# First stage in nine groups of tokens, three of 256 and six of 384; the lead needs two blocks of 128; idle products in the lead

## What is computed

```python
for t in range(S):                                   # stage 0, S = 768, D = 48
    cur = np.einsum('bhd,bhe->bhde', u[None] * kt, vt)
    y[:, :, t] = np.einsum('bhd,bhde->bhe', rt, state + cur)
    state = wt[:, :, :, None] * state + np.einsum('bhd,bhe->bhde', kt, vt)
...
h = x @ w_in                                         # first dense stage, 384 -> 2048 -> 384
g = np.where(pos, h, np.where(neg, 0.0, (h + beta) ** 2 / (4.0 * beta)))
x = g @ w_out
...
silu = g * (1.0 / (1.0 + np.exp(-g)))                # second dense stage, 384 -> 1536 -> 384
out = silu * (x @ w_val) @ w_out
```

## Time and profile before

| | us |
|---|---|
| median of 3 runs | 966.13 (965.5 to 968.37) |
| profiled execution, its time | 966.24 |
| its span, first to last instruction | 964.5 |
| PE busy (9142 products) | 947.0 |
| DVE busy | 519.5 |
| ACT busy | 402.5 |
| POOL busy | 164.2 |

### The profile page before, as it was taken

The page is one execution under the profiler, slowest core; times in us unless marked ns, Lnnn a source line. Parts: engine busy times, 40 slices in busy tenths (PEclk is TensorE's granted clock), DMA queues, the critical chain, the costliest instruction groups (busy, mean ns, idle before and its releaser), DMA issues.

```text
span 964.5 us, 22023 instructions
## 1 busy us (share of the span) xinstructions
PE 947.0 (98%) x9142; PEld 928.7 (96%) x9142; DVE 519.5 (54%) x909; ACT 402.5 (42%) x845; POOL 164.2 (17%) x155
## 2 busy tenths in 40 slices
PE   6899999999999999999999999999999999999998
...
DMA packets 23511, 61.96 MB, mean 64 GB/s; under 512 B 2688, under 2 KB 12032, under 8 KB 23424
## 3 DMA queue, kind: packets, MB, share of 16 engines
...
## 4 chain that ended last, share of the span: by engine, by line
PE 94%; DVE 3%; issue 1%; ACT 1%; DMA 1%; SPq 0%; DVEq 0%; ACTq 0%
PE bank L1254 50%; PE bank L1282 35%; PE bank L1313 2%; PE bank L1337 2%; PE bank L1332 2%; PE bank L1302 1%; PE bank L1343 1%; DMA w_by_channel<-in_w_channel 1%; PE bank L1324 1%; DVE suf L1000 1%; DVE gate L1104 0%; DVE glo L1097 0%; DVE k_r_by_channel L1025 0%; PE bank L1299 0%; ACT state_decayed L806 0%
## 5 line engine op out<-in xcount | busy, mean ns | idle before, releaser
L841 ACT ACTIVATE ghi<-gate 128x384 fp32r<-128x384 f32 x224 | 117.2, 523 | 184.9 <-DVE gate L1116 95.4
L1097 DVE TENSOR_TENSOR glo<-gate,ghi 128x384 fp32r<-128x384 f32 x224 | 133.5, 596 | 106.3 <-ACT ghi L841 104.0
L1114 DVE TENSOR_TENSOR gate<-bank,gate 128x384 f32<-128x384 f32 x96 | 53.5, 558 | 215.0 <-ACT gate L960 215.0
L1254 PE MATMUL bank<-xhi,w2gv_ahi 128*128 128x384 f32 x480 | 161.3, 336 | 0.0
L1254 PE MATMUL bank<-xlo,w2gv_ahi 128*128 128x384 f32 x480 | 161.3, 336 | 0.0
L1254 PE MATMUL bank<-xhi,w2gv_alo 128*128 128x384 f32 x480 | 161.3, 336 | 0.0
L960 ACT ACTIVATE gate<-bank 128x384 f32<-128x384 f32 x96 | 47.2, 492 | 227.7 <-PE bank L1254 227.7
L1282 PE MATMUL bank<-ghi,w1ohi 128*128 128x384 f32 x384 | 133.9, 349 | 0.9 <-DVE glo L1097 0.9
L1254 PE MATMUL bank<-xhi,w1ihi 128*128 128x384 f32 x384 | 129.2, 337 | 2.1 <-DVE gate L1104 1.2
L1282 PE MATMUL bank<-glo,w1ohi 128*128 128x384 f32 x384 | 129.2, 336 | 0.0
L1254 PE MATMUL bank<-xhi,w1ilo 128*128 128x384 f32 x384 | 129.1, 336 | 0.0
...
## 6 DMA issues: line engine op xcount, KB each, us to landing
...
```

The source lines that it names most:

```text
L841: e.activation(ghi[j % 2][:, :], gate[j % 2][:, :], ACT.Copy).then_inc(M["hi", ph], 1)
L1097: e.tensor_tensor(glo[j % 2][:, :], gate[j % 2][:, :], ghi[j % 2][:, :].bitcast(F32), ALU.subtract)\
L1114: e.tensor_tensor(q, hid[j % 2][:, 0:T], q, ALU.mult).then_inc(M["t", 2], 1)
L1254: m = e.matmul(out, w_of(a, k), x_of(b_, k), start=start and i == 0, stop=stop and i == total - 1)
```

## The change

The first stage is worked in nine groups: three of two windows (256 tokens), then six of three (384 tokens). The second stage keeps its eight groups of 384. In the first three groups, each product of the first stage has 256 columns instead of 384, and so have the gate's instructions on ACT and DVE; the number of products in a group stays at 288. The lead has two windows instead of three; the third window's pieces move into the slots of group 0. Groups of two windows have slot tables of their own, and windows are counted through from 0 to 23, so the three buffers of r, k, v and w are used in turn over group borders. The transfers of the lead stand in another order: window 2's come behind the first weight chunks. DVE forms the rests of seven chunks (0, 1, 3, 7, 13, 19, 25) instead of one. In the lead, idle products of 128x256 stand in PE's list (five ahead of KT of window 0, on a tile of zeros; three on constants ahead of KT of window 1, three ahead of Y of window 0) in place of the twelve transposes. The result of a group of 256 is stored in one or two pieces.

```diff
+SIZES = (2, 2, 2, 3, 3, 3, 3, 3, 3)
+NG1 = len(SIZES)
+BASE = [sum(SIZES[:g]) for g in range(NG1 + 1)]
+ROW = S // WIN
+PIECES = 6
...
 FIRST_FILLS = [("KT", 0, 0), ("AT", 0, 0), ("AT", 0, 1), ("ST", 0, 0),
                ("KT", 1, 0), ("AT", 1, 0), ("AT", 1, 1), ("Y", 0, 0),
-               ("ST", 1, 0), ("KT", 2, 0), ("AT", 2, 0), ("AT", 2, 1),
-               ("Y", 1, 0), ("Y", 2, 0), ("XT", 0, 0), ("XT", 1, 0), ("XT", 2, 0), ("ST", 2, 0)]
-
-WARM = 12
+               ("Y", 1, 0), ("XT", 0, 0), ("XT", 1, 0), ("ST", 1, 0)]
+FIRST_BANKS = (0, 1, 2, 3, 4, 5, 6, 7, 0, 1, 3, 2)
+IDLE = {("KT", 0): 5, ("KT", 1): 3, ("Y", 0): 3}
+
...
-XT_FIRST = 13
+
+
+def visits_at(n, slots):
+    return {j: tuple(FILLS[n].index(f) for f in visit) for j, visit in zip(slots, VISITS[n])}
+
+
+WIN_SLOTS = {2: visits_at(2, (3, 5, 7, 9, 11)), 3: visits_at(3, (3, 5, 6, 8, 9, 11, 12))}
+WIN_FIRST = visits_at(2, (4, 6, 8, 10, 12))
+XT_FIRST = 12
...
-CHECK_FIRST = {0: 1, 3: 2}
-SCAN_FIRST = {1: 1, 5: 2}
-SCALE_FIRST = {0: 0, 2: 1, 8: 2}
-DIAG_FIRST = {2: 0, 5: 1, 7: 2}
-SCAN_SLOTS_FIRST = {11: 0, 14: 1, 15: 2}
-
-
-DVE_CHUNK = 3
+CHECK_FIRST = {0: 1}
+SCAN_FIRST = {1: 1}
+SCALE_FIRST = {0: 0, 2: 1}
+DIAG_FIRST = {3: 0, 7: 1}
+SCAN_SLOTS_FIRST = {11: 0, 14: 1}
+
+
+DVE_CHUNKS = (0, 1, 3, 7, 13, 19, 25)
+DVE_CHUNK_SLOTS = {1: 7, 4: 13, 7: 19, 10: 25}
 HI_FIRST = {0: 13, 1: 13, 2: 15, 3: 18, 4: 21, 5: 24, 6: 27, 7: 30, 8: 32}
-PRODUCTS_AT = {10: 0, 17: 1, 22: 2}
-VALUES_AT = {16: 0, 23: 1, 28: 2}
+PRODUCTS_AT = {5: 0, 14: 1}
+VALUES_AT = {12: 0, 20: 1}
 
...
+def no(g, w):
+    return BASE[g] + w
+
+
+def place_of(n):
+    g = max(g for g in range(NG1) if BASE[g] <= n)
+    return g, n - BASE[g]
+
+
 def win_slots(g):
-    return WIN_FIRST if first(g) else WIN_SLOTS
+    return WIN_FIRST if first(g) else WIN_SLOTS[SIZES[g + 1]]
...
+        def width(ph, g):
+            return T if ph == 2 else SIZES[g] * WIN
...
+            load_w(1)
             e.dma_start(cst[:, :], cst_d).then_inc(ld["cst"], 16)
-            load_kr(0, 1)
-            load_tok(0, 0)
+            load_tok(0)
+            load_kr(1)
             e.dma_start(uu[:, :], u_d).then_inc(ld["u"], 16)
-            load_w(0, 2)
-            load_kr(0, 2)
-            load_tok(0, 1)
-            load_w1(1)
-            load_tok(0, 2)
-            load_w1(RING - 1)
-            load_w(1, 0)
-            load_kr(1, 0)
-            load_w(1, 1)
-            load_tok(1, 0)
+            load_tok(1)
             load_w1(4)
-            load_kr(1, 1)
-            load_w(1, 2)
-            load_tok(1, 1)
-            load_w1(4)
-            load_kr(1, 2)
-            load_tok(1, 2)
+            load_w(2)
+            load_w1(2)
+            load_kr(2)
+            load_w1(2)
+            load_tok(2)
+            load_w1(RING - 8)
+            load_w(3)
+            load_kr(3)
+            load_tok(3)
             load_w1(2 * J1)
-            for w in range(NW):
-                load_w(2, w)
...
             def drain_at(w):
-                for n in range(2):
-                    drain(0, fill_no(0, "AT", w, n), 0)
-
-            for w in range(2):
-                scan_window(0, w)
-                scale_window(0, w)
-            diag_sum(0, 0)
+                for i in range(2):
+                    drain(0, fill_no(0, "AT", w, i), 1)
+
+            for n in range(SIZES[0]):
+                scan_window(n)
+                scale_window(n)
             drain_at(0)
-            scan_window(0, 2)
-            scale_window(0, 2)
+            diag_sum(0)
             drain_at(1)
-            drain(0, fill_no(0, "ST", 1), 0)
-            diag_sum(0, 1)
-            diag_sum(0, 2)
-            drain_at(2)
+            diag_sum(1)
+            w1_lo(0)
+            w1_lo(1)
             for kind in ("Y", "XT"):
-                for w in range(NW):
-                    drain(0, fill_no(0, kind, w), 0)
-            drain(0, fill_no(0, "ST", 2), 0)
-            w1_lo(DVE_CHUNK)
-            suffix_scan(1, 0)
+                for w in range(SIZES[0]):
+                    drain(0, fill_no(0, kind, w), 1)
+            drain(0, fill_no(0, "ST", 1), 1)
+            w1_lo(3)
+            suffix_scan(no(1, 0))
             knee(0, 0)
             lo(1, 0, 0)
             knee(0, 1)
-            prefix_scan(1, 0)
+            prefix_scan(no(1, 0))
             sum_w(0)
...
+                    if j in DVE_CHUNK_SLOTS:
+                        w1_lo(DVE_CHUNK_SLOTS[j])
...
+            def idle(ahead_of):
+
+                for _ in range(IDLE.get(ahead_of, 0)):
+                    if ahead_of == ("KT", 0):
+                        e.wait_ge(zero_p, 5)
+                        zero = att[0][0]
+                        e.matmul(acc[2][:, 0:2 * WIN], zero[:, 0, :], zero[:, 0:2, :].rearrange("p a t -> p (a t)"), start=True, stop=True)
+                    else:
+                        e.matmul(acc[2][:, 0:2 * WIN], ident, cst[:, 0:2 * WIN], start=True, stop=True)
...
-                products(hid[j % 2][:, 0:T], lambda a, k: w1i[a][:, j, k * P:(k + 1) * P],
-                         lambda b_, k: xs[b_][:, k, :], KT, True, True).then_inc(M["h", 1], 1)
+                t = width(1, g)
+                products(hid[j % 2][:, 0:t], lambda a, k: w1i[a][:, j, k * P:(k + 1) * P],
+                         lambda b_, k: xs[b_][:, k, 0:t], KT, True, True).then_inc(M["h", 1], 1)
```

More of the change, by code:

```diff
@@ L119, in fills, with fill_done, piece_done, stores_ahead @@
 def fills(g):
-    return FIRST_FILLS if first(g) else FILLS
+    return FIRST_FILLS if first(g) else FILLS[SIZES[g]]
 def fill_no(g, kind, w, n=0):
     return fills(g).index((kind, w, n))
+def fill_done(g, f):
+    return PIECES * BASE[g] + f + 1
+def piece_done(n, kind):
+    g, w = place_of(n)
+    return fill_done(g, fill_no(g, kind, w))
+def stores_ahead(g):
+    return sum(len(x2_pieces(i)) for i in range(g))
+def x2_pieces(g):
+    pieces, t = [], BASE[g] * WIN
+    while t < BASE[g + 1] * WIN:
+        end = min(BASE[g + 1] * WIN, (t // T + 1) * T)
+        pieces.append((t // T, t % T, t - BASE[g] * WIN, end - t))
+        t = end
+    return pieces
 def build_program(nc, w_d, kr_d, tok_d, u_d, cst_d, w1i_d, w1o_d, w2g_d, w2v_d,
@@ L628, in half @@
                 if after_next:
-                    for w in range(NW):
-                        if g > 0:
-                            load_w(g + 2, w)
-                    for w in range(NW):
-                        load_kr(g + 2, w)
-                        load_tok(g + 2, w)
+                    windows = range(BASE[g + 2], BASE[g + 3])
+                    if g > 0:
+                        for n in windows:
+                            load_w(n)
+                    for n in windows:
+                        load_kr(n)
+                        load_tok(n)
@@ L839, in hi @@
                 if ph == 2 and isinstance(g, int) and g == 0 and j < 2:
-                    e.wait_ge(M["out", 1], (NG + 1) * J1 - 1 + j)
-                e.activation(ghi[j % 2][:, :], gate[j % 2][:, :], ACT.Copy).then_inc(M["hi", ph], 1)
+                    e.wait_ge(M["out", 1], (NG1 + 1) * J1 - 1 + j)
+                t = width(ph, g)
+                e.activation(ghi[j % 2][:, 0:t], gate[j % 2][:, 0:t], ACT.Copy).then_inc(M["hi", ph], 1)
             def knee(g, j):
@@ L899, in slot @@
             def slot(g, j, parity, next_half, after_next):
-                last = isinstance(g, int) and g == NG - 1
+                last = g == NG1 - 1
                 finished, started = nxt(g, j + 1, J1), nxt(g, j + 2, J1)
@@ L1297, in do_fill @@
                         e.wait_ge(ld["cst"], 16)
-                    for _ in range(WARM if first(g) and w == 2 else 0):
-                        e.transpose(out[:, 0:P], ident, ident)
-                    e.wait_ge(scaled, 2 * (g * NW + w) + 1)
+                    e.wait_ge(scaled, 2 * n + 1)
                     for p in range(NPAIR):
-                        m = e.transpose(out[:, p * PR:(p + 1) * PR], kr[:, w, 0, p, :], ident[0:PR, 0:PR])
+                        m = e.transpose(out[:, p * PR:(p + 1) * PR], kr[:, s, 0, p, :], ident[0:PR, 0:PR])
                 elif kind == "AT":
@@ L1348, in bank_free @@
                 if first(g):
-                    gg, ff = 0, f - 8
-                    if ff < 0:
+                    earlier = [i for i in range(f) if FIRST_BANKS[i] == FIRST_BANKS[f]]
+                    if not earlier:
                         return
+                    gg, ff = 0, earlier[-1]
                 elif f >= NBANK:
```

446 lines of the change are left out of this document (215 added, 231 removed), and 17 rows, old and new, of the table VISITS.

## The result

The changed kernel takes 978.56 us (median of 4 runs, 978.2 to 979.31), the kernel before 966.39 beside it (4 runs, 965.5 to 968.37). The ratio is 1.0130, with a 95% interval of 1.0117 to 1.0143: slower by 12 us. Forecast was slower by 6.6.

A forecast was written before the change was run, and what follows sets the result against it. PE bounds all groups but the first, where DVE is nearly full too; DVE is the full engine in the lead. -7.2 + 4.8 + 3.7 + 2.7 + 2.6 = +6.6 on 966.24 gives 972.8 us, range 961 to 980.

The forecast's parts named there:

- slot 0 starts earlier: In the lead, DVE's shorter list lets slot 0 start at 26.2 us, 7.2 us earlier; bounds 24.7 to 27.7.
- products: On PE after slot 0's start, 846 products of 256 columns at 120 ns and 1728 of 384: 4.8 us more.
- third window of the lead, now in slots: On PE after slot 0's start, the pieces of the lead's third window are done in slots: 3.7 us more.
- waits in group 0 and what hangs on them: In group 0, PE's slots shrink but DVE's work per window does not: 2.7 us more waiting, bounds 0 to 8.
- the same at the borders of groups 1 and 2: Scans in slots 13 and 14 make the third lo late, 1.3 us for each group: 2.6 us more, bounds 0 to 5.
- the late lead: Rival, 10%: POOL's chain for window 1 or ACT's first chunks hold the lead; slot 0 4 us earlier, not 7: 976.
- The rival in which only columns count: Rival, 18%: a product of 256 columns takes 108 ns on PE, total 962.7 us; decided below 109 ns.
- that of the weight loads: Rival, 6%: weight loads bound the narrow product on PE at 140 ns, total 989.7 us.
- a third more products: By the skill's formula 256 columns take 109.2 ns on PE, so a third more products would cost almost nothing.
- Waits of group 0, slots 0 to 3: DVE's lo, done at 30.3, 33.4 and 38.6 us, make PE wait 4.9 us in all, against 2.2 before after slot 0.
- Waits of group 0 behind slot 3: After slot 3, fills lengthen PE's slots, DVE has no more work than PE, POOL is ahead by 2 us or more.

The follow-up runs named there:

- e2: The changed kernel without the three idle products ahead of Y, the other eight kept: 978.76 us, ratio 1.0129 to the kernel before.
- e5: The changed kernel without any of its eleven idle products: 979.55 us, ratio 1.0135 to the kernel before.
- e1: The changed kernel with POOL's diag_values placed behind chunks 16 and 26, not 12 and 20: 974.89 us, ratio 1.0084 to the kernel before.
- e8: e1 plus, in narrow groups 1 and 2, scans of group g+2's windows in slots 10, 12, 14 instead of 10, 13, 14: 973.45 us, ratio 1.0079.
- e3: The changed kernel with fifteen idle products added between the first two tile_in and slot 0: 983.74 us, ratio 1.0181 to the kernel before.
- e6: e1 with the first scan of group 1 behind the gates of steps 0 and 1 on DVE: 975.61 us, ratio 1.0101.
- e12: The changed kernel with four idle products added ahead of slot 0: 979.21 us, ratio 1.0133 to the kernel before.
- e4: The changed kernel with the rest of chunk 7 moved from DVE's slot 1 back to POOL: 978.34 us, ratio 1.0120 to the kernel before.
- e9: The changed kernel with the edits of e1 and e8 and the rest of chunk 7 on POOL: 971.72 us, ratio 1.0056 to the kernel before.
- e11: e9 with group 1's second-window scans and scalings later (slots 3, 5) and group 2's scans in group 0's slots 10, 13, not 11, 14: 973.43 us, ratio 1.0071.

## Why the direction was right and half of the size was missing

The span grew by 13.0 us. By the forecast's own terms:

| term | forecast | measured |
|---|---|---|
| slot 0 starts earlier | -7.2 | -5.9 |
| products | +4.8 | +3.1 |
| third window of the lead, now in slots | +3.7 | +3.7 |
| waits in group 0 and what hangs on them | +2.7 | +9.1 |
| the same at the borders of groups 1 and 2 | +2.6 | +3.0 |
| sum | +6.6 | +13.0 |

The 9.1 lies outside the forecast's own bounds for that term, 0 to 8; the total stayed in the range because its upper end, 980, had been set by another rival, the late lead. That is luck.

**The lead.** `tile_in` began at 23.25 and slot 0 at 27.46, for 22.1 and 26.2. AT of window 0 took 1.16 us at 7.90, not 2.08, as the five idle products were meant to do. AT of window 1 took 2.03, since the clock had fallen again; it doesn't matter (e2, e5). But a single trace doesn't fix this term to better than 1 us. In e1 and e8, whose instructions up to here are the same, slot 0 starts at 27.61 and 25.77. And e3, e6 and e12 show that the start of slot 0 was the wrong thing to count: what passes on of it is only what DVE's list up to slot 3 lets through.

**The products.** 118 ns for the 120 forecast: 846 x 0.118 + 299.5 - 396.2 = 3.1. The excess over the columns is 13.3 ns at 384 and 11 at 256: between a fixed cost, which the forecast took (13.3 again, 120 ns), and one that grows with the columns (8.9, 115.6 ns, its bound). So the term was 1.7 us too large. The rival in which only columns count (under 109 ns) is out, and so is that of the weight loads (140). The Trainium skill (TensorE: Matmul & The Clock Gate, Back-to-back issue gap) gives N/2.4 + 2.5 ns as the gap of an isolated product, an estimate of 109.2 ns for 256 columns, and says that in a stream with weight loads both operations set the distance. The prediction carried the formula over to a stream without that condition; the measurement decides for 118. (The prediction's "a third more products" is also off: over the first 768 tokens they go from 576 to 864, half more.)

**The third window: right.** In group 1 the same product stands at 83.17 and 126.88, 43.71 us apart. Without 1.70 us of waits, twice 0.27 and 288 x 0.118 = 34.0, 7.5 are left for two windows, 3.7 each.

**Waits of group 0, slots 0 to 3: right in what sets them, too long by 0.9 us, and on time partly by luck.** DVE in order of time, ahead of slot 3:

```profile
37.94 0.53 DVE L1159 TENSOR_TENSOR w1olo<-ring_b,w1ohi 128x384 fp32r<-128x384 f32 x1
38.39 0.42 DVE L1120 TENSOR_TENSOR glo<-gate,ghi 128x256 fp32r<-128x256 f32 x1
```

The `lo` were done at 31.3, 34.5 and 38.8, for 30.3, 33.4 and 38.6. The first two were 1.0 and 1.1 us late, since slot 0 was 1.3 late; the third caught up, because the interval before it was 4.3 us and not 5.2: the chunk's rest took 0.5 of DVE's time and not 1.1. From slot 0 to `tile_out` of slot 3 it was 11.5 us for 12.4. Idle time was 1.91 us, for 4.9 (which the times given in the prediction add up to only 4.5, 0.7 + 0.8 + 2.9 and 0.1). Most of what is missing was filled by the half clock of slot 0, which took 1.6 us more for its 18 products (31.23 - 27.46 = 3.77 us for 2.12). Where the clock was full (e2), 3.1 us.

**Waits of group 0 behind slot 3: the step that failed.** "After slot 3 [...] POOL's 25 rests and six diag instructions at 1.3 us are 40 us from 19 on, ahead of need by 2 us or more." I counted POOL's work and not its order. The change put `diag_values` behind chunk 12 (16 before) and moved `diag_sum` to DVE's slots 3 and 7 (2 and 5 before); there POOL waits, and with it all later chunk rests. What each part measured: two waits for POOL, 3.47 us; the half clock that follows the first (48.10 to 51.50), 1.5, since nine products and the 32 behind them took 2.26 and 1.30 us for 1.30 and 0.80; two waits behind group 0's own scans in slots 11 and 14, 1.50, which I had counted for groups 1 and 2 and forgotten here. e1 shows the first two together: without them the time falls by 4.5 us by the ratios, 5.0 worked out (2 x 0.27 would come on top, as told next, and the wait at slot 3 that grew by 0.8 goes off). The two are not tied, though: in e4 the same wait for POOL (2.08 us, until 48.97) is followed by no half clock (granted 1.00 from 48.9 to 60.0).

**A cost that no step had.** Each wait ahead of products costs 0.27 us more than its idle time, as worked out above. There are eight of them after slot 0's start, one before: 1.9 us.

Group 0 has 1.91 + 3.47 + 1.50 = 6.88 us of idle time less 2.16 of before, 1.6 + 1.5 of half clock, 4 x 0.27 = 1.1, and 0.2 for a stop at slot 2 too short for the list above (0.39 us between the starts at 34.28 and 34.67): 9.1. The borders have 2.18 + 3 x 0.27 = 3.0. That the sum meets the span so closely is partly luck, since each half clock stretch is known to a few tenths only.

**Waits in groups 1 and 2.** The first border has 1.70 us (1.3 forecast), the second 0.48 (1.3): group 2's last slots already have `tile_in` of 384 columns behind them, which the step had overlooked. That the scans in slots 13 and 14 make them, e8 shows by half, in its trace and not in its time.

**What stays open.** Why the clock fell where it did. That PE had stood idle shortly before each time is all that is seen: ahead of 48 us it had been busy 4.13 of 6 us. The place differs from trace to trace. e2, e6 and e8 have a stretch of half clock behind the wait of slot 3 (1.92, 2.25 and 2.75 us), the changed kernel, with 1.91 us there, has not; e9 has waits too, and its slots ran at full clock. Where such a stretch falls is worth some 1.5 us, as much as most differences between the experiments; of the steps from one kernel to the next only e1's 4.5 and e3's 4.9 us are well above it. e4 and e11 are within what the comparison can tell.
